# Four token tiles of 512 and two of 480 in place of five of 512 and one of 448

## What is computed

```python
qn = q / (norm(q, axis=tokens) + 1e-6)          # q, k, v: (1, 6016, 256)
kn = k / (norm(k, axis=tokens) + 1e-6)
a  = softmax(kn.transpose(0, 2, 1) @ qn / tau)  # (256, 256)
x  = v @ a                                      # (6016, 256)
h  = x @ w_in1;  x = (h - tanh(h)) @ w_out1     # 256 -> 2048 -> 256
h  = x @ w_in2;  g = where(h > 0, h, exp(min(h, 0)) - 1)
out = g @ w_out2                                # (6016, 256)
```

## Time and profile before

| | |
|---|---|
| median of three runs | 1030.37 us (1030.22 to 1030.6) |
| the profiled execution, its own time | 1030.58 us |
| its span in the profile | 1028.8 us |
| TensorE busy with matmuls | 1023.7 us, 4574 matmuls |
| weight loads | 858.6 us |
| VectorE busy | 821.3 us |
| ScalarE busy | 767.2 us |
| TensorE's granted clock, mean | 0.999 of full speed |

### The profile page before, as it was taken

The page is one execution under the profiler, slowest core; times in us unless marked ns, Lnnn a source line. Parts: engine busy times, 40 slices in busy tenths (PEclk is TensorE's granted clock), DMA queues, the critical chain, the costliest instruction groups (busy, mean ns, idle before and its releaser), DMA issues.

```text
span 1028.8 us, 13741 instructions
## 1 busy us (share of the span) xinstructions
PE 1023.7 (100%) x4574; PEld 858.6 (83%) x4574; DVE 821.3 (80%) x1362; ACT 767.2 (75%) x1360; POOL 0.8 (0%) x7
## 2 busy tenths in 40 slices
PE   9999999999999999999999999999999999999998
PEld 8868888888888888888998888888888888888997
DVE  5899977777867776777999888887887887887876
ACT  6687776666766666767778878778778787878775
POOL 0000000000000000000000000000000000000000
PEclk9999999999999999999999999999999999999999
DMA  9932002003003001012212002102101201200202
GB/s 354 302 70 41 1 31 52 1 22 62 1 9 70 0 1 42 1 41 72 62 54 96 1 1 62 21 1 56 26 1 42 42 1 37 42 1 1 41 1 36
DMA packets 117830, 46.24 MB, mean 45 GB/s; under 512 B 100352, under 2 KB 108544, under 8 KB 117760
## 3 DMA queue, kind: packets, MB, share of 16 engines
q1 hardware_dynamic: 113616, 43.99, 16.0%
q10 hardware_dynamic: 4144, 1.38, 0.5%
HBM read 33.03 MB, written 12.32 MB: 44 GB/s over the span
## 4 chain that ended last, share of the span: by engine, by line
PE 98%; DVE 1%; issue 0%; DMA 0%; ACT 0%; POOL 0%; DVEq 0%; POOLq 0%
PE r_ps L327 16%; PE r_ps L326 16%; PE r_ps L328 16%; PE x_ps L327 6%; PE x_ps L328 6%; PE x_ps L326 6%; PE z_ps L328 4%; PE z_ps L327 4%; PE z_ps L326 4%; PE y_ps L327 2%; PE q_ps L327 2%; PE y_ps L328 2%; PE q_ps L326 2%; PE q_ps L328 2%; PE y_ps L326 2%; PE x_ps L333 2%
## 5 line engine op out<-in xcount | busy, mean ns | idle before, releaser
L606 ACT ACTIVATE g_hi<-g 128x512 fp32r<-128x512 f32 (+1 forms) x384 | 236.2, 616 | 137.4 <-DVE g L854 54.7
L707 DVE TENSOR_TENSOR g_lo<-g,g_hi 128x512 fp32r<-128x512 f32 (+1 forms) x384 | 259.6, 677 | 49.6 <-ACT g_hi L606 40.8
L326 PE MATMUL r_ps<-g_hi,w_out_hi 128*128 128x512 f32 (+1 forms) x768 | 296.1, 385 | 0.0
L328 PE MATMUL r_ps<-g_hi,w_out_lo 128*128 128x512 f32 (+1 forms) x768 | 295.7, 385 | 0.0
L327 PE MATMUL r_ps<-g_lo,w_out_hi 128*128 128x512 f32 (+1 forms) x768 | 295.7, 385 | 0.0
L326 PEld LDWEIGHTS r_ps<-g_hi,w_out_hi 128*128 128x128 f32 x768 | 144.2, 188 | 27.5 <-DVE g_lo L707 0.6
L328 PEld LDWEIGHTS r_ps<-g_hi,w_out_lo 128*128 128x128 f32 x768 | 144.2, 188 | 26.8
L327 PEld LDWEIGHTS r_ps<-g_lo,w_out_hi 128*128 128x128 f32 x768 | 144.2, 188 | 26.6
L326 PE MATMUL x_ps<-t_hi,w_ops 128*128 128x512 f32 (+1 forms) x288 | 111.4, 387 | 0.0
L327 PE MATMUL x_ps<-t_lo,w_ops 128*128 128x512 f32 (+1 forms) x288 | 111.0, 385 | 0.0
L328 PE MATMUL x_ps<-t_hi,w_ops 128*128 128x512 f32 (+1 forms) x288 | 110.9, 385 | 0.0
(11 more groups left out here) (109 smaller groups left out, 1485.0 us busy)
## 6 DMA issues: line engine op xcount, KB each, us to landing
v_blocks<-v_dram SPq DMA_DIRECT2D x40, 128.0 KB, 3.0
x_scratch<-side SPq DMA_DIRECT2D x20, 256.0 KB, 2.0
vt<-x_scratch SPq DMA_DIRECT2D x20, 256.0 KB, 3.5
out_dram<-v_blocks SPq DMA_DIRECT2D x80, 64.0 KB, 1.9
k_ring<-k_dram SPq DMA_DIRECT2D x9, 512.0 KB, 10.1
q_ring<-q_dram SPq DMA_DIRECT2D x9, 512.0 KB, 10.9
w_out_raw<-moe_w_out_dram SPq DMA_DIRECT2D x1, 2048.0 KB, 15.2
w_raw<-moe_w_in_dram SPq DMA_DIRECT2D x16, 128.0 KB, 2.5
```

The lines of the kernel that those rows point to most:

```text
L326: nc.tensor.matmul(ps, w_hi, m_hi, start=start, stop=False, skip_group_check=True)
L328: return nc.tensor.matmul(ps, w_lo, m_hi, start=False, stop=stop, skip_group_check=True)
L606: nc.scalar.activation(g_hi[b][n % DEPTH[b]][:, 0:width], g[b][:, 0:width], ACT.Copy).then_inc(g_rounded[b], 1)
L707: return nc.vector.tensor_tensor(lo, x, hi.bitcast(F32), ALU.subtract)
```

## The change

One line. The two last pairs get 480 columns each, in both networks; the number of pairs, quads and matmuls and the sum of the widths stay. No other line differs, and each engine has the same instructions in the same order, with other widths in pairs 4 and 5.

```diff
 TILE = 512
-WIDTH = [512] * 5 + [448]
+WIDTH = [512] * 4 + [480] * 2
 PAIRS = len(WIDTH)
 TOKEN0 = [2 * sum(WIDTH[:p]) for p in range(PAIRS)]
```

## The result

The changed kernel takes 1033.47 us, the median of 20 runs (1032.88 to 1035.97), against 1030.63 us for the kernel before in 20 runs beside them. The ratio is **1.0029, with a 95% interval of 1.0023 to 1.0035**: the change makes the kernel slower, by 3.0 us by the ratio and 2.8 us by the medians. The forecast was 1031.5 us and no change that can be told; the time lies in the stated range, and on the side of the third rival. The range was nearly as wide as the rivals together, 1027.6 to 1035.6, so lying in it says little; the forecast of no change that can be told did not come true.

A forecast was written before the change was run, and what follows sets the result against it. TensorE's start-to-start matmul time was taken to bound the kernel. 1440 matmuls at 215.4 ns (+1.1 us) and the tail (+0.1) made +1.2 us on the 1030.37 us median: 1031.5 us, range 1027.6 to 1035.6.

The forecast's parts named there:

- the third rival: Pairs 4 and 5: every matmul of 480 stays out of step, ending over 0.2% slower, 1032.8 to 1036.3 us; chance 0.30.
- out of step: Pairs 4 and 5: matmuls of 480 don't fall into a rhythm as 512 does; a quad takes 9.72 us and above.
- the term T: Start-to-start cost of one matmul of 480 columns in pairs 4 and 5, 1440 of them; forecast 215.4 ns.
- the by-column value: T for pairs 4 and 5, by columns between 448 and 512: 214.67 ns, sum 309.12 us, no change.
- the mixed stretch: Border of pairs 4 and 5, six matmuls of 512 interleaved with six of 448: 216.2 ns each, 2.3 us more.
- the edge of slower: Pairs 4 and 5: from T = 216.03 ns on, the time is more than 0.2% up.
- the fixed rule: Every TensorE matmul: columns over 2.4 GHz plus a fixed 2.5 ns, by the Trainium skill; change worth 0.0 us.
- the rhythm: TensorE: equal matmuls of 512 fall into a lower cost, 13.33 ns beyond columns, lost for some starts when width changes.
- The 2.7 ns: f32 score matmuls of 256 columns on TensorE: 216 ns apart, read as 2.7 ns above what 512 columns take.
- The tail: After TensorE's last matmul: one transpose, last stores and VectorE's and ScalarE's chain grow, 0.1 us more.

The follow-up runs named there:

- the scan: Kernel replaced by a plain series of f32r matmuls, 60 of each width, no other engine at work: 226.67 ns at 512, 216.67 at 480, 202.67 at 448.
- all twelve entries of the series: Plain series, no kernel: forty f32r matmuls per width, each behind one of twelve other widths; 480 at 216.67 ns, 512 at 226.67, 448 at 202.67 or 206.67.

## Why the prediction was right or wrong

**Right: what bounds the kernel, and where to look.** TensorE's start-to-start time was the one thing that the change moved. The rest came as forecast: pairs of 512 at 10.20, no pause on TensorE in pairs 4 and 5 before the last quad, VectorE and ScalarE hidden. The quad times that it listed (9.60, 9.66, 9.69, 9.72 and above) tell the cases apart, and 9.75 is the last of them, out of step.

**Wrong: the term T.** The sum was right in form, 1440 T against 309.12 us. The step that failed is "I take halfway between the by-column value and the mixed stretch: 215.4 ns". It measured 216.67, so 1.8 us were missing, and 216.03 was the edge of slower. With 216.67 the same sum gives 2.88 + 0.1 = 2.98 us more, against 2.84 between the medians. Two things were in the halving that no row carried. The by-column value treats the cost beyond the columns as straight between two widths, and the scan shows that it isn't: 13.33 at 512 and 16.67 at each of 504, 496, 488, 480 and 472. The two neighbours were the low point and a middling one. And the mixed stretch, 216.2, was shaved because a pure stretch "has more chance to settle than a mixed one". It did settle, behind all twelve entries of the series, and the place where it settled was dear. That the mixed stretch lies within 0.5 ns of the result is luck, though. Its starts show that it isn't a stretch of 480 in any sense: in each round the six matmuls of 512 take (467.45 - 466.07) / 6 = 230 ns each, 3.4 above their steady cost, and the six of 448 take 202.2, close to their steady 202.67. What it priced is the disturbed 512 at a border.

**The third rival** had the right place, the right direction and a price of 2.3 us at 216.2, with a chance of 0.30. Its words "never settled" were wrong: 480 is steady, at its own cost.

**Right: the weight of the fixed rule.** The forecast said that the Trainium skill's fixed 2.5 ns doesn't cover f32r, and that the change would be worth 0.0 us by it. In the series it is exact for bf16 and off by 9 to 17.5 ns for f32r. My leaning towards weight loads as the reason for the rhythm is half answered: with a quarter of the weight columns the time beyond the columns stays, but the low cost goes over from 512 to 480. The 2.7 ns that the prediction read for the f32 scores is a rounding; their starts are 215.84 ns apart, 2.5 ns beyond 512 columns.

**The tail** was +0.1 us forecast. The piece after the last matmul's start grew by 0.18, the wait before it shrank by 0.1; 0.1 in all. The argument that VectorE's chain there would grow more than TensorE's matmuls came out the other way. Matmuls of 480 grew by 14.0 ns each and not by 12, which by the prediction's own count of 20 matmuls is 0.04 us of it; the rest wasn't measured. So the 0.1 us came out right as a sum of two parts of which one had the wrong sign.

**Open.** Why the f32r stream has these steady costs, why they go by the first column read in 64 columns, and what decides between the two costs of 448, isn't settled by any run. The runs leave out the other engines and the number of rows from 64 up; the weight columns don't set the size of the cost but change which width has which. The PSUM side, and strides between tiles other than 512 and 1024 columns, weren't tried.

## What to carry to other kernels

When TensorE is the bound, price a change of tile width from start-to-start times of exactly that width, in a series of forty or more matmuls of the same data type, and then in the kernel, since 448 had 202.67 ns in one series and one network and 206.67 in others; a line through two other widths can miss by more than the change is worth. Splits of the same columns into the same number of matmuls aren't equal: here 512 and 448 cost 429.3 ns together and twice 480 costs 433.3. And before widths are shuffled, try where the operand begins in its buffer, which costs nothing; here it helped the 448 columns, and neither 512 nor, by more than 0.67 ns, 480.

## What the runs showed of the hardware

- A matmul over f32r data costs 11.8 to 20.0 ns beyond its columns at full clock (256 to 512 columns, start at 0 or shifted), one over bf16 2.5 ns, with the same 128 weight columns.
- At the 1.2 GHz level an f32r matmul of 512 columns costs its columns alone, 426.67 ns, with 32 rows and with 128.
- With 32 weight columns in place of 128, 480 has 13.33 ns beyond its columns and 512 has 18.40, where they had 16.67 and 13.33.
- The same matmul has several steady costs: 448 columns at 202.67 or 206.67 ns from column 0. The dearer one lasted for some 220 matmuls in one kernel, until two late starts, and in another it began in the middle of an unbroken stretch and lasted for some 130.
- The first column read moves the steady cost: 448 from 200.00 (column 16) to 206.67 (column 8), 512 from 226.67 (0 and 64) to 233.37 (8).
- With operands of 32 rows the granted clock fell to 0.50, the 1.2 GHz level, in the middle of an unbroken series, and came back when 128 rows were used again.
